# Keys turned by whole-array transposes, and round 0 of the recurrence spread over eight PSUM banks

## What is computed

```python
# stage 1, for every batch and head: a recurrence over the 768 tokens
y[t]  = r[t] @ (state + (u * k[t])[:, None] * v[t][None, :])
state = w[t][:, None] * state + k[t][:, None] * v[t][None, :]
# stage 2, x = y as 3072 tokens of 384
x = ((x @ w_a) * (x @ w_b)) @ w_out          # inner width 1536
# stage 3
h = x @ w_in                                  # inner width 2048
out = (max(h, 0) + alpha * min(h, 0)) @ w_out2
```

## Time and profile before

| what | value |
|---|---|
| median of three runs | 1023.63 us |
| the profiled execution, its own time | 1024.34 us |
| its span on the engines | 1022.5 us |
| TensorE matmul (PE) busy | 1000.7 us, 98% |
| TensorE weight loads (PEld) busy | 976.0 us, 95% |
| DVE busy | 559.5 us, 55% |
| ACT busy | 288.7 us, 28% |
| POOL busy | 24.4 us, 2% |
| data moved by DMA | 53.01 MB |

### The profile page before, as it was taken

One profiled execution on the slowest core, in us unless ns is written; L12 is line 12 of the kernel. 1 busy time (PEld: TensorE's weight loads), 2 busy tenths in 40 slices (PEclk: granted clock), 3 DMA queues, 4 the chain that ended last, 5 costly groups with the idle time before them and its releaser, 6 DMA issues.

```text
span 1022.5 us, 29089 instructions
## 1 busy us (share of the span) xinstructions
PE 1000.7 (98%) x12448; PEld 976.0 (95%) x12448; DVE 559.5 (55%) x1170; ACT 288.7 (28%) x604; POOL 24.4 (2%) x24
## 2 busy tenths in 40 slices
PE   5799999999999999999999999999999999999998
PEld 5799999999999999999999999999999999999998
DVE  7487664655656646556432437645455554545554
ACT  3435314223232242241222434222222212122212
POOL 4400000000000000000000000000000000000000
PEclk9999999999999999999999999999999999999999
DMA  6554311411213013010020313010101010101000
GB/s 159 140 156 113 87 55 30 114 29 47 69 30 91 25 30 92 15 52 25 25 60 1 114 58 124 1 47 1 47 1 47 1 46 0 46 0 47 10 15 24
DMA packets 42167, 53.01 MB, mean 52 GB/s; under 512 B 5184, under 2 KB 42048, under 8 KB 42048
## 3 DMA queue, kind: packets, MB, share of 16 engines
q1 hardware_dynamic: 40624, 51.04, 17.5%
q10 hardware_dynamic: 1424, 0.23, 0.1%
HBM read 39.46 MB, written 9.44 MB: 48 GB/s over the span
## 4 chain that ended last, share of the span: by engine, by line
PE 96%; DVE 1%; issue 1%; ACT 0%; DMA 0%; ACTq 0%; DVEq 0%; SPq 0%
PE products L166 18%; PE products L167 16%; PE products L168 16%; PE acc L168 12%; PE acc L166 11%; PE acc L167 11%; PE products L696 5%; PE products L711 1%; PE products L740 1%; PE products L756 1%; PE products L673 1%; PE products L725 1%; DMA x_parts<-f_y 0%; DVE k_in L931 0%; DVE a_sb L948 0%
## 5 line engine op out<-in xcount | busy, mean ns | idle before, releaser
L166 PE MATMUL products<-x_parts,weights_hi 128*128 128x384 f32 x576 | 201.0, 349 | 3.6 <-DMA x_parts<-f_y 1.5
L167 PE MATMUL products<-x_parts,weights_hi 128*128 128x384 f32 x576 | 194.2, 337 | 0.0
L168 PE MATMUL products<-x_parts,weights_lo 128*128 128x384 f32 x576 | 193.9, 337 | 0.0
L1239 DVE TENSOR_SCALAR leaky_low<-products,leaky_al 128x384 f32<-128x384 f32 x128 | 79.0, 617 | 169.6 <-PE products L168 169.5
L1099 DVE TENSOR_TENSOR g_sb<-a_g,products 128x384 f32<-128x384 f32 x96 | 53.2, 554 | 195.4 <-issue 133.1
L1186 ACT ACTIVATE leaky_g_hi<-leaky_g_sb 128x384 fp32r<-128x384 f32 x128 | 67.3, 525 | 295.0 <-DVE leaky_g_sb L1244 295.0
L514 ACT ACTIVATE g_hi<-g_sb 128x384 fp32r<-128x384 f32 x96 | 50.3, 524 | 255.0 <-DVE g_sb L1099 255.0
L166 PEld LDWEIGHTS products<-x_parts,weights_hi 128*128 128x128 f32 x576 | 108.1, 188 | 8.9 <-issue 5.0
L168 PEld LDWEIGHTS products<-x_parts,weights_lo 128*128 128x128 f32 x576 | 108.2, 188 | 0.0
L167 PEld LDWEIGHTS products<-x_parts,weights_hi 128*128 128x128 f32 x576 | 108.2, 188 | 0.0
L168 PE MATMUL acc<-g_hi,weights_lo 128*128 128x384 f32 x288 | 97.5, 338 | 0.0
(11 more groups left out here) (85 smaller groups left out, 1754.9 us busy)
## 6 DMA issues: line engine op xcount, KB each, us to landing
k_in<-in_k_dram SPq DMA_DIRECT2D x16, 336.0 KB, 4.2
r_in<-in_r_dram SPq DMA_DIRECT2D x16, 336.0 KB, 5.2
stage<-in_w_out_dram SPq DMA_DIRECT2D x14, 384.0 KB, 3.2
w_v<-in_v_dram SPq DMA_DIRECT2D x16, 288.0 KB, 3.8
y_dram<-x_in SPq DMA_DIRECT2D x8, 576.0 KB, 3.0
x_in<-y_dram SPq DMA_DIRECT2D x8, 576.0 KB, 4.6
out_dram<-leaky_out_sb SPq DMA_DIRECT2D x7, 576.0 KB, 3.3
stage<-in_w_dram SPq DMA_DIRECT2D x10, 336.0 KB, 3.8
```

Source lines behind the costliest of these rows:

```text
L166: pe.matmul(out, w_hi, x_hi, start=first, stop=False)
L167: pe.matmul(out, w_hi, x_lo, start=False, stop=False)
L168: return pe.matmul(out, w_lo, x_hi, start=False, stop=last)
L1239: dve.tensor_scalar(self.low[f % 2][:, :], h, 0.0, self.al[:, f:f + 1], ALU.min, ALU.mult).then_inc(self.low_ready, 1)
```

## The change

All of it but the turning of the keys concerns round 0, phase 0 of round 1 and the first steps of stage 2.

- `turn_keys` transposes 112 by 128 of `k_in` at once, six instructions for each stream in place of 24, in all rounds. `copy_kt` reads the new layout.
- In round 0 levels 3 and 5, the second stream's turned keys, key-value products and outputs go to banks that were idle (`acc0` to `acc2`, `products` bank 4), so no stage waits there for the one before it to be read. `weighted_values` of both streams stand ahead of the wait for the states.
- In round 0 `last_step_k` goes from POOL to DVE, and DVE steps the keys of a level before it merges the level before.
- The outputs of the second stream of round 0 are copied and lowered in four parts of 48 rows, where there were two of 112. ACT prepares the next round's keys between and behind its output copies, where it did so ahead of them. All six moves now wait for the first stream's outputs alone; SP issues five, ACT one.
- Pieces 3 and 4: SP loads them behind the moves and the two loads of `w` for round 1; ACT rounds them within steps 0 and 1 of stage 2; POOL subtracts them after that.
- Two groups of matmuls whose results nothing reads are added: three between the first and the second stream's state products, five between the two leaves of round 1.

```diff
-HI_AT = [2, 3, 4, BEFORE_TILES, 11]
-BETWEEN_OUTPUTS = 3
+HI_AT = [2, 3, 4]
 LO_AT = [7, 8, 9, 9, 11]
-LOAD_AT = [7, 8, 11, 11, 11]
+LOAD_AT = [11, 11, 11, 11, 11]
...
+            def level_ps(n, phase, hd):
+
+                if n == 0 and phase == 3:
+                    return acc[hd], 0
+                if n == 0 and phase == 5:
+                    return (products, 4 * BANK) if hd == 0 else (acc[2], 0)
+                return products, BANK * (2 * ((phase + (n == 0 and phase == 4)) % 2) + hd)
...
+            def key_values_ps(n, j, par):
+
+                if n > 0:
+                    return products, stream_bank(j, par)
+                return (products, BANK * (2 + par)) if j == 0 else ((products, 4 * BANK), (acc[2], 0))[par]
+
+            def outputs_ps(n, j, par):
+
+                return (acc[par], 0) if n == 0 and j == 1 else (products, stream_bank(j, par))
...
                     elif phase == 10:
                         copy_outputs(n, 0)
                         if n == 0:
-                            shared.split_hi(act, BETWEEN_OUTPUTS)
+                            prepare_k(n + 1, 0)
+                            act.wait_ge(lowered, outputs_lowered(n, 3))
+                            move_rows(act, n, KT - 1, 64)
                         copy_outputs(n, 1)
                         if n == 0:
-                            act.wait_ge(lowered, outputs_lowered(n, OUTPUTS - 1))
-                            for q in range(1, KT):
-                                move_rows(act, n, q, 64)
+                            prepare_k(n + 1, 1)
...
                     copy(a_g[:, :], a_ps).then_inc(a_copied, 1)
+                    if g == 1:
+                        shared.split_hi(act, EARLY - 1)
                     if g > 0 and step_at(g - 1) is not None:
                         attend_late(step_at(g - 1))
                     act.wait_ge(g_ready, g + 1)
                     act.wait_ge(down_done, from0(g - 1))
                     copy(g_hi[f % 2][:, :], g_sb[:, :]).then_inc(g_hi_ready, 1)
+                    if g == 0:
+                        shared.split_hi(act, EARLY - 2)
...
                     for c in range(CH):
-                        for hd in range(2):
-                            for par in range(2):
-                                last = pe.matmul(view(products, stream_bank(j, hd) + D * c, [[1, D]], BLOCK, BLOCK * par),
-                                                 key_blocks(k_in[j], hd, c, par), ident[64 * hd:64 * hd + D, :], start=True, stop=True)
+                        tile, at = keys_ps(n, j, c // HALF)
+                        at += ROWS * (c % HALF)
+                        last = pe.transpose(tile[:, at:at + ROWS], k_in[j][:, c * P:(c + 1) * P], ident[:, :])
                     last.then_inc(products_done[j], 1)
...
+                def unread_products(count):
+
+                    pe.wait_ge(shared.w_hi_ready, 1)
+                    for _ in range(count):
+                        w_hi, _ = shared.parts("w_a", 0, 0, TT)
+                        pe.matmul(products[:, 2 * BANK:2 * BANK + TT], w_hi[:, 0:P], w_hi, start=True, stop=True)
+
                 def outputs(n):
 
                     if n == 0:
                         for j in range(2):
                             if j == 1:
-                                weighted_values(n, j)
+                                unread_products(3)
+                            pe.wait_ge(states_done[j], states_after(n))
...
                         leaf(n, 0)
+                        if n == 1:
+                            unread_products(5)
                         leaf(n, 1)
```

More of the change, by code:

```diff
@@ L186, in merges, with parts_of, parts_before @@
     return 12 * duo + (0 if phase == 0 else 2 * phase + 2) + part + 1
+def parts_of(duo):
+    return OUTPUTS if duo else FIRST_OUTPUTS
+def parts_before(duo):
+    return FIRST_OUTPUTS + OUTPUTS * (duo - 1) if duo else 0
 def copies(duo, what, j, side):
-    return (5 + OUTPUTS) * duo + (0 if what == "level" else 1 + 2 * j) + side + 1
+    before = 5 * duo + parts_before(duo)
+    if what == "level":
+        return before + (1 if duo else 3)
+    return before + (2 * j + side + 2 if duo or j else side + 1)
 def outputs_copied(duo, part):
-    return (5 + OUTPUTS) * duo + 5 + part + 1
+    return 5 * duo + parts_before(duo) + 5 + part + 1
 def outputs_lowered(duo, part):
-    return OUTPUTS * duo + part + 1
+    return parts_before(duo) + part + 1
 def states_after(duo):
@@ L325, in leaf_ps @@
             def leaf_ps(n, j, hd):
-                return (acc[hd], 0) if n <= 1 and j == 1 else (products, stream_bank(j, hd))
+                return (acc[hd], 0) if n == 0 and j == 1 else (products, stream_bank(j, hd))
+            def key_values_ps(n, j, par):
[4 more added lines that the diff above has]
+                return (acc[par], 0) if n == 0 and j == 1 else (products, stream_bank(j, par))
             def output_parts(n):
@@ L553, in copy_kt @@
                     act.wait_ge(products_done[j], after(n, 6))
-                    for hd in range(2):
-                        copy(view(k_scratch[j], D * CH * hd, [[1, D * CH]], P),
-                             view(products, stream_bank(j, hd), [[1, D * CH]], P)).then_inc(copied, 1)
+                    for unit in range(2):
+                        tile, at = keys_ps(n, j, unit)
+                        copy(view(k_scratch[j], D * HALF * unit, [[D, HALF], [D * CH, 2], [1, D]], P),
+                             view(tile, at, [[ROWS, HALF], [64, 2], [1, D]], P)).then_inc(copied, 1)
                 def copy_outputs(n, stream):
@@ L593, in attend_late @@
                     elif phase == 9 and 0 < n and n + 1 < DUOS:
-                        prepare_k(n + 1, 1)
-                    elif phase == 9 and n == 0:
-                        prepare_k(n + 1, 0)
                         prepare_k(n + 1, 1)
@@ L622, in _ @@
                 prepare_r(0, 1)
-                for hd in range(2):
-                    rows = slice(64 * hd, 64 * hd + 64)
-                    act.dma_start(ident[rows, :], constants[rows, 64 * hd:64 * hd + D]).then_inc(ident_loaded, 16)
+                act.dma_start(ident[:, :], constants[0:ROWS, 0:ROWS]).then_inc(ident_loaded, 16)
                 for step in range(BEFORE_TILES):
@@ L700, in turn_keys @@
                 def turn_keys(n, j):
-                    if j == 0:
+                    if n == 0:
+                        pe.wait_ge(merged, merges(0, 2 + j, 1))
+                    elif j == 0:
                         pe.wait_ge(merged, merges(n, 4, 1))
@@ L719, in key_values @@
                     pe.wait_ge(copied, copies(n, "keys", j, 1))
+                    if n == 0 and j == 0:
+                        pe.wait_ge(merged, merges(0, 4, 1))
+                    elif n == 0:
+                        pe.wait_ge(copied, copies(0, "level", 0, 0))
+                        pe.wait_ge(last_level_copied, 1)
                     pe.wait_ge(v_loaded[j], 16 * (n + 1))
@@ L796, in attend @@
                         key_values(n, 0)
+                        if n == 0:
+                            weighted_values(n, 0)
                     elif phase == 9:
                         key_values(n, 1)
-                        weighted_values(n, 0)
+                        weighted_values(n, 0 if n else 1)
                     elif phase == 10:
@@ L816, in wait_x @@
                 def wait_x(tile, kt):
-                    part = 3 if kt == 0 else OUTPUTS - 1
+                    part = 3 if kt == 0 else parts_of(tile) - 1
                     pe.wait_ge(copied, outputs_copied(tile, part))
```

118 lines of the change are left out of this document (72 added, 46 removed).

## The result

The changed kernel takes **1026.43 us** (median of 12 runs, 1023.43 to 1029.91), the kernel before 1023.13 (12 runs on the same chip, 1022.01 to 1025.67). The ratio is 1.0029, 95% interval 1.0016 to 1.0041: slower by 0.3%. That is inside the range of the forecast, 2.1 us above its number, and on the side to which it gave 0.20. The profiled execution of the changed kernel is its slowest: its own time is 1029.91, 3.5 us above the median, its span 1028.1. So what it shows is larger than in a typical run. The spread of the runs is part of the result: 6.5 us against 3.7 before. Of all runs behind this document one took 1216.86 us (a run of experiment 7, at a granted clock of 0.76); it is left out of that kernel's ratio.

What follows compares the result with a forecast made beforehand. TensorE's list was taken as the bound, with DVE's chain arriving without slack at `down` of step 1. Head -2.8, DVE held +3.5 and transposes 0 gave +0.7, from 1023.63 to 1024.3 us; whole range 1020.0 to 1026.8.

Steps and rivals of the forecast that it cites:

- rival D: Head of the kernel: instruction stream falls behind again, outputs come no earlier, DVE still held; +3.0, 1026.6 us; chance 0.07.
- Same: Whole kernel: time within 0.2% of the kernel before, 1021.6 to 1025.7 us; chance 0.49.
- The transposes: Turning of keys, rounds 1 to 7: 12 transposes take 1.54 us like 48 matmuls, change 0; bounds -6.6 and +10.7 us.
- The head: Round 0 up to the first step of stage 2: step 1 comes 2.8 us earlier; bounds 1.4 and 3.6.
- the unread matmuls cost nothing: Head: the eight unread matmuls lie in existing waits and cost nothing; without that cover 1.4 us.
- Pieces 3 and 4: Round 1's keys and queries scaling: POOL's late subtractions hold DVE, +3.5 us; bounds 0 and 3.7.
- Step 2 needs both by 53.3 and is not held up by them: Step 2 of stage 2: both late weight pieces are subtracted by 53.3 us, so it does not wait.
- Rival A: Stage 2's early steps: POOL does not hold DVE, so the head's gain stays; 1020.8 us; chance 0.30.
- C: Turning of keys: a transpose costs as two full instructions, 10.7 us more, 1035 us; chance 0.05.
- B: Head: TensorE's clock rises late, state products and leaves run slow, costing 1.4 of the gain; 1025.7 us; chance 0.13.
- No later gap in which to win it back: From 49.69 to 57.57 us: what delays DVE delays the kernel one for one; TensorE cannot recover it later.
- The last sentence of the forecast: Around `down` of step 1: mechanism wrong if TensorE waits for something else, such as pieces 3 to 8, 3 us later.

Runs made afterwards that it cites:

- experiment 7: The kernel before with the whole-array transposes alone, plus two POOL subtractions during DVE's stretch, their results overwritten later; median 1021.13 us.
- experiment 8: The changed kernel with bulk loads issued behind the weight pieces, but without the eight unread matmuls; median 1024.34 us.
- experiment 4: The kernel before with nothing but the whole-array transposes, `copy_kt`'s layout and the larger identity; median 1018.46 us.
- experiment 1: The changed kernel, with SP issuing the loads of values and queries at step 1 behind that step's weight pieces; median 1022.05 us.
- experiment 3: The changed kernel with pieces 3 and 4 loaded early, in round 0, and rounded ahead of the first step of stage 2; median 1019.0 us.
- experiment 10: Experiment 3 with the second `prepare_k` ahead of ACT's copies of the second stream's outputs; median 1018.48 us.
- experiment 6: Experiment 4 plus ten unread matmuls behind the two leaves of round 1; median 1018.46 us.
- experiment 11: Experiment 3 with old output copies, `prepare_k` order and moves, and eight unread matmuls behind round 1's leaves, none between them; median 1020.25 us.

## Why the prediction was right, and where it was not

**The number.** 1024.3 was forecast, 1026.43 measured, inside 1020.0 to 1026.8. That it came this near is in part luck, because what the sum missed lies on both sides: the transposes below, the hole and the lower clock behind it above. The nearest number is rival D's 1026.6, and that is chance: D had the outputs come no earlier, and they came 3.9 us earlier (36.10 against 39.98). "Same" had 0.49 and the result is slower by 0.29%, so the likeliest case was not the one that came.

**The transposes: mis-sized.** I took 0, "the nearest row". A transpose takes 90 ns at the upper level (1.08 us for 12 in round 1, granted clock 1.00), is recorded once, and gives 0.46 us a round, 3.2 in seven. The nearest row was that of small matmuls which fill the array four at a time, and I carried its time for a load over to an instruction of another kind; between bounds of -6.6 and +10.7 the value was a guess in the form of a row. The Trainium skill, TensorE: Matmul & The Clock Gate, LDWEIGHTS, led to 107 ns and -1.8; the trace is lower, 90, and the rule's direction was right where I saw no change. Its other rule (PE-mode transpose: a transpose does not count as busy for the clock) did not decide anything here: with the transposes the upper pace is reached ahead of the state products, where it was not before, and behind the turning of round 1 (98.99 on) the large matmuls keep their 0.17 us.

**The head: right, slightly short.** -2.8 forecast, -3.37 measured in step 1's start. The gap in the turning is gone, the state products start at 34.72 (34.7 forecast), the copy came at 36.10 (37.0 forecast), the first step at 42.83 (43.3), with no pause at its second third. The 37.0 is not what its terms give: 39.98 - 2.8 + 0.2 is 37.4. The copy is earlier than either because the state products took 1.33 us and not the old 2.44, the case that the forecast had only as its upper bound. The sentence that the unread matmuls cost nothing stands, but it missed their worth: without them the kernel loses 2.3 (experiment 8). The transposes alone also start step 1 2.17 us early (47.49, experiment 4), so that much of the head's gain does not need the rest of the change. With the fault in the queue mended, the rest of the change together loses 3.6 against the transposes alone (experiment 1 against 4); mended further it breaks even (experiments 3 and 10).

**Pieces 3 and 4: the mechanism right, one sentence wrong.** DVE was held 3.04 us (3.5 forecast), in its products of decays. `down` of step 1 came at 57.30 for 58.5, because the head brought more and the hold took less. "Step 2 needs both by 53.3 and is not held up by them" failed: ACT could round piece 4 only at 52.25 (50.6 forecast), since SP took 4.34 us for its six issues where I had 2.8; piece 3 was rounded at 49.66 and not from 48.0, 3.5 us behind its last issue where I had 1.6; POOL subtracted piece 4 from 53.18, and TensorE stood 2.22 us for it. That cost nothing beyond DVE's hold, which runs beside it; it is also why the wait for `g_lo` is only 0.42 us where the forecast named about 3. Rival A fell in experiment 7, C by the single record of each transpose, B by the pace of the state products and leaves. D fell on its main count, the outputs, though an "issue" gap of 1.22 us did come back ahead of the state products.

**The step that failed** is the one I had not taken: the sum ended at `down` of step 1. "No later gap in which to win it back" was true, and I read it as if nothing could be lost later either. Pieces 5 to 8 and the bulk loads go through the same queue as pieces 3 and 4, and shifting two pieces behind the moves shifts them all. The last sentence of the forecast names "pieces 3 to 8, which now come 3 us later" as what would break it, but gives it no term, no rival and no price. Its price was 4.4 us of the median (experiment 1). In the profiled run, the slowest, it was 9.6: 5.7 for the hole and 3.9 for the 9.3 us at the lower clock behind it. The parts seen in the profiles (-0.5 at `down`, -3.2 for the transposes, +4.4) give +0.7 and the medians differ by 3.3, so some 2.6 us of a typical run stays unexplained; granted clocks under 1.000 in runs that were not profiled are where I would look.

## What to carry to other kernels

When a load is moved later in a queue, follow everything behind it until the queue has caught up, and ask of each item in which engine's list its consumer stands: here bulk loads that nobody was waiting for, put ahead of one small piece, stopped an in-order engine in front of the 0.47 us copy that TensorE needed. Price a stall on TensorE together with the clock behind it, which in the one execution profiled cost two thirds as much again. And time the parts of a bundle singly: one part of this one gives 0.5%, the whole loses 0.3%.

## What the runs showed of the hardware that was not expected

- A float32 transpose of 112 by 128 takes 90 ns at the upper level in a row of 12, and 218 to 222 ns in round 0 (1.31 to 1.33 us for six), where the matmuls around it run at about half their later pace though the granted clock reads 1.00. That is a ratio of 2.4, more than the factor of 2 between the levels.
- One DMA of 384 KB took 9.18 us to land behind four loads, and at most 3.4 in experiment 1 without them in front.
- "Issue" gaps of 0.66 to 2.49 us on TensorE end 1.2 to 1.7 us after a 16 KB packet of its instruction queue has landed, nineteen of nineteen. The DMA share inside them ranges from 0.00 to full, so busy DMA engines are not what they need.
- Eight matmuls that nobody reads, 1.9 us of TensorE's time, are worth 2.3 us where they keep the clock up; ten or eight in another place (experiments 6 and 11) are worth nothing on the total, and both profiles show a stretch at the lower level ahead of them.
